# Another order of loads, transposes and vector work around the two halves of an attention stage, before two MLPs

## The reference

```python
B, H, S, D = q.shape                          # 2, 8, 768, 64; block 32, window 16
k_sum = k.reshape(B, H, nb, block, D).max(axis=3)
v_sum = v.reshape(B, H, nb, block, D).mean(axis=3)
scores_l = scale * q @ k^T, kept where |i - j| < window
scores_s = scale * q @ k_sum^T + log(block)
a = softmax over both together
x = a @ concat(v, v_sum)                      # to 1536 tokens x 512
xn = x / rms(x) * rms_g
x = (silu(xn @ w_gate) * (xn @ w_val)) @ w_out     # 512 -> 1536 -> 512
h = x @ w_in ; out = (h - tanh(h)) @ w_out2        # 512 -> 2048 -> 512
```

## Time and profile before

| | us |
|---|---|
| median of 3 runs | 628.69 (628.62 to 629.18) |
| the profiled execution, its own time | 630.96 |
| its span, first to last instruction | 628.9 |
| PE busy in it | 612.5 |
| DVE, ACT, POOL busy | 428.5, 324.1, 171.3 |
| mean granted TensorE clock | 0.995 of full |

### The profile page before, as it was taken

One profiled execution on the slowest core, in us unless ns is written; L12 is line 12 of the kernel. 1 busy time (PEld: TensorE's weight loads), 2 busy tenths in 40 slices (PEclk: granted clock), 3 DMA queues, 4 the chain that ended last, 5 costly groups with the idle time before them and its releaser, 6 DMA issues.

```text
span 628.9 us, 10726 instructions
## 1 busy us (share of the span) xinstructions
PE 612.5 (97%) x3990; PEld 570.6 (91%) x3990; DVE 428.5 (68%) x699; ACT 324.1 (52%) x622; POOL 171.3 (27%) x223
## 2 busy tenths in 40 slices
PE   7889799999999999999999999999999999999997
PEld 7669699999999998889898899999999989898986
DVE  4798567567753449877777689999543597666643
ACT  5676254444433327555555467776332375555542
POOL 4673512021210303322220545662200222222200
PEclk9999989999999999999999999999999999999999
DMA  9998913312311121222222162222323023222102
GB/s 257 189 242 152 185 51 93 92 35 60 93 51 51 52 68 50 69 74 65 75 63 68 45 200 67 68 68 77 91 57 112 0 73 96 67 68 68 33 2 100
DMA packets 96210, 53.90 MB, mean 86 GB/s; under 512 B 33760, under 2 KB 90336, under 8 KB 95968
## 3 DMA queue, kind: packets, MB, share of 16 engines
q1 hardware_dynamic: 95728, 52.44, 32.2%
q10 hardware_dynamic: 432, 0.79, 0.3%
HBM read 50.07 MB, written 3.15 MB: 85 GB/s over the span
## 4 chain that ended last, share of the span: by engine, by line
PE 86%; SPq 10%; DVE 2%; DMA 1%; issue 1%; ACT 1%; DVEq 0%
PE bank L931 11%; PE bank L935 11%; PE bank L933 11%; PE bank L874 10%; PE bank L876 10%; PE bank L875 10%; PE bank L1040 7%; PE bank L1039 7%; PE bank L1038 7%; SPq L497 4%; SPq L447 2%; PE bank L858 1%; PE bank L809 1%; DMA x_raw<-in_moe_w_gate_dram 1%; PE bank L838 1%
## 5 line engine op out<-in xcount | busy, mean ns | idle before, releaser
L1700 DVE TENSOR_TENSOR h_lo<-pd,h_hi 128x384 fp32r<-128x384 f32 x112 | 70.2, 628 | 28.9 <-ACT h_hi L1426 13.9
L1040 PE MATMUL bank<-y_hi,h_lo 128*128 128x512 f32 x192 | 75.5, 393 | 0.0
L1039 PE MATMUL bank<-y_lo,h_hi 128*128 128x512 f32 x192 | 75.4, 393 | 0.0
L1038 PE MATMUL bank<-y_hi,h_hi 128*128 128x512 f32 x192 | 75.3, 392 | 0.0
L698 POOL TENSOR_TENSOR ws_raw<-x_raw 128x256 f32<-128x256 f32 x16 | 12.0, 752 | 209.0 <-PE bank L935 127.5
L874 PE MATMUL bank<-h_hi,z_hi 128*128 128x384 f32 x192 | 64.9, 338 | 0.0
L876 PE MATMUL bank<-h_hi,z_lo 128*128 128x384 f32 x192 | 64.5, 336 | 0.0
L875 PE MATMUL bank<-h_lo,z_hi 128*128 128x384 f32 x192 | 64.5, 336 | 0.0
L1293 ACT CAST h_hi<-pd 128x384 fp32r<-128x384 f32 x48 | 24.8, 516 | 45.5 <-DVE pd L1730 33.6
L1410 ACT COPY part<-bank 128x384 f32<-128x384 f32 x48 | 23.0, 479 | 43.3 <-PE bank L935 42.2
L1040 PEld LDWEIGHTS bank<-y_hi,h_lo 128*128 128x128 f32 x192 | 36.0, 188 | 8.2
(11 more groups left out here) (207 smaller groups left out, 1727.6 us busy)
## 6 DMA issues: line engine op xcount, KB each, us to landing
x_raw<-in_moe_w_in_dram SPq DMA_DIRECT2D x32, 256.0 KB, 3.4
y_raw<-in_moe_w_out_dram SPq DMA_DIRECT2D x32, 256.0 KB, 2.8
x_raw<-in_moe_w_gate_dram SPq DMA_DIRECT2D x24, 256.0 KB, 3.3
y_raw<-in_moe_w_val_dram SPq DMA_DIRECT2D x24, 256.0 KB, 3.3
z_raw<-in_moe_w_out_dram SPq DMA_DIRECT2D x16, 384.0 KB, 3.5
k_rows<-in_k_dram SPq DMA_DIRECT2D x8, 384.0 KB, 5.6
qn<-in_q_dram SPq DMA_DIRECT2D x12, 256.0 KB, 7.1
vw_early<-in_v_dram SPq DMA_DIRECT2D x12, 192.0 KB, 6.1
```

Of the source, the lines that this page charges most:

```text
L1038: nc.tensor.matmul(AB[t][:], a_hi, w_hi, start=begins, stop=False, skip_group_check=True)
L1039: nc.tensor.matmul(AB[t][:], a_hi, w_lo, start=False, stop=False, skip_group_check=True)
L1040: last = nc.tensor.matmul(AB[t][:], a_lo, w_hi, start=False, stop=ends, skip_group_check=True)
L1700: nc.vector.tensor_tensor(dst, full, high.bitcast(f32), ALU.subtract).then_inc(done, 1)
```

## The change

1. **Load queue.** Gate and value columns 2 and 3 (`load_xy(2)`, `load_xy(3)`) and values of tiles 6 and 7 are issued among the queries of batch 1; the two loads of z follow after them.
2. **`blk`.** The 96 rows are numbered by block first, head pair second, and are loaded in two transfers (one for each head of the pairs, 96 partitions with a row of 8 KB) instead of four (one for each pair, 24 partitions with two rows). `gather_sums` takes every fourth column of the identity instead of 24 neighbouring ones.
3. **Tile 0.** On PE `transpose_probs(0, 0)` comes before the three block-sum steps, `transpose_probs(0, 1)` before the third. On ACT each `copy_probs(0, par)` follows its `exp(0, par)`, ahead of the first `means`.
4. **Tile 6.** On DVE `copy_q1(4)` comes before the loop (behind `low_h(0,1,1)`) instead of after `gated(0,2,0)`, and `shift(6, 0)` before `product(0,2,0)` instead of after `low_h(0,2,0)`.

```diff
-    v_b = v.rearrange("b (c h) (n t) d -> b c n h (t d)", h=2, t=BLOCK)
+    v_b = v.rearrange("b (c h) (n t) d -> b h n c (t d)", h=2, t=BLOCK)
...
             sp.wait_ge(means_mm, 1)
-            for c in range(KC):
-                sp.dma_start(blk[c * NBLK:(c + 1) * NBLK, :, :], v_b[1, c]).then_inc(blk_in, 16)
-            for t in range(1, TPB):
-                load_q(TPB + t)
+            for hf in range(2):
+                sp.dma_start(blk[:, hf, :], v_b[1, hf]).then_inc(blk_in, 16)
+            load_q(TPB + 1)
+            load_q(TPB + 2)
+            load_xy(2)
+            load_q(TPB + 3)
+            load_xy(3)
+            load_q(TPB + 4)
+            load_q(TPB + 5)
+            load_values(TPB)
+            load_values(TPB + 1)
             for m in range(2):
                 load_z(m)
-            for i in range(J1 // 2):
-                if i:
-                    load_xy(2 * i)
-                    load_xy(2 * i + 1)
+            for i in range(2, J1 // 2):
+                load_xy(2 * i)
+                load_xy(2 * i + 1)
                 load_values(TPB + i)
...
-            pool.wait_ge(blk_in, 16 * KC)
+            pool.wait_ge(blk_in, 32)
...
-                                            ident[0:KC * NBLK, c * NBLK:(c + 1) * NBLK],
+                                            ident[0:KC * NBLK, c:KC * NBLK:KC],
...
             scores(1)
-            block_sums()
+            transpose_probs(0, 0)
+            block_sums(0)
+            block_sums(1)
+            transpose_probs(0, 1)
+            block_sums(2)
...
             exp(0, 0)
+            copy_probs(0, 0)
             exp(0, 1)
+            copy_probs(0, 1)
             act.wait_ge(means_mm, 1)
             means(vw_early[:, 0], TX).then_inc(means_act, 1)
             copy_q(2)
-            copy_probs(0, 0)
-            copy_probs(0, 1)
...
             low_h(0, 1, 1)
+            copy_q1(4)
...
                 if T == TPB:
-                    copy_q1(4)
+                    shift(T, 0)
                     product(0, j, 0)
                     dve.wait_ge(half_added, ADDS)
                     low_h(0, j, 0)
-                    shift(T, 0)
                     shift(T, 1)
```

More of the change, by code:

```diff
@@ L813, in scores, with block_sums @@
                 last.then_inc(scored, 1)
[L815 to L821, removed]
+            def block_sums(m):
+                if m == 0:
+                    pe.wait_ge(ind_done, 1)
+                pe.wait_ge(v_paired, m + 1)
+                last = nc.tensor.matmul(TX[WIN:KEYS, :], ind[:, m, :], v_rows[:, :, 2 * m * D:(2 * m + 1) * D],
+                                        start=m == 0, stop=m == ROWS // 2 - 1)
+                if m == ROWS // 2 - 1:
+                    last.then_inc(means_mm, 1)
             def gather_sums():
@@ L1127, in _ @@
                     gate(0, 0, 0)
-                transpose_probs(T, 0)
-                transpose_probs(T, 1)
+                if T:
+                    transpose_probs(T, 0)
+                    transpose_probs(T, 1)
                 if T >= 2:
```

## The result

| | before | after |
|---|---|---|
| median | 628.62 (626.82 to 629.18, 5 runs) | 624.05 (623.86 to 624.33, 5 runs) |
| ratio | | 0.9943, interval 0.9922 to 0.9964 |
| profiled execution: time, span | 630.96, 628.9 | 624.17, 622.0 |
| mean granted clock in it | 0.995 | 0.999 |

The kernel is faster, by 4.6 us from median to median. Between the two profiled executions it is 6.9 us of span. The time lies inside the range, near its upper end; the forecast was 7.1 us of gain, less 0.1 for small waits, and 621.7 us.

A forecast was written before the change was run, and what follows sets the result against it. PE was taken as the bound, pausing between batches behind gate column 2's late landing. 6.96 us there plus 0.15 from the first stage made 7.1; 628.69 less that, plus 0.1 for small waits, gave 621.7 us, range 620.3 to 625.0.

The forecast's parts named there:

- The cause: Passage between batches: late gate column 2 delays ACT's split and key copies, DVE's maxima and `copy_q1(3)`, so PE waits 3.56 us.
- The sum: Whole kernel: 6.96 us from the passage plus 0.15 from the first stage, 7.1 us gained.
- The lower clock's part: PE from `gather_sums` to `transpose_probs(6, 0)`: 2.78 us of the 6.96 gain, from the clock staying at full speed.
- the gain taken over whole gives 628.69 - 7.1 = 621.6: Whole kernel: full gain from the profiled execution subtracted from the median of runs, before 0.1 us for small waits.
- the last sentence of the prediction: Least sure: whether unprofiled runs have the whole pause; if the 2.27 us difference lies in it, gain 4.8, time 623.9.
- The range's lower end: Whole kernel: 620.3 us, from the full 0.65 us of the first stage and a `scores(6)` at half.
- POOL in DVE's way: Rival, 0.06: POOL's earlier additions at 53 to 64 us slow DVE, passage some 1 us later, 622.7 us.
- the shorter pause: Rival, 0.14: passage between batches, PE still stops 1 to 2 us and the clock falls, 624.4 to 625.9 us.
- doesn't do what it says: Rival, 0.05: load queue, column 2 still lands after 70 us, the pause stays, 628.2 us.
- the slower case: Rival, 0.05: `blk` lands late and PE stops at `gather_sums`; at half drain rate 11 us later, 639 us.

The follow-up runs named there:

- the two holds: Kernel after, columns 2 and 3 held until batch 1's third query tile is transposed, or until `gate(0,1,1)` is done: 629.75 and 630.36 us.
- The 99 executions: The kernel before, unchanged, timed over five sets: 625.79 to 633.27 us.

## Where the prediction was right, and which step failed

**The cause was right.** The late column, the wait of ACT, the key copies, the maxima, `copy_q1(3)` and PE's pause stood in the forecast as a chain, and the two holds show it as a cause: with the column late again, the pause and the time are back.

**The sum was right for the execution that it was read from.** 630.96 - 7.1 = 623.9 was forecast for it, and the profiled execution after took 624.17. Between the spans are 6.9 us. The first stage and `gather_sums` gave 0.55 us (its end at 70.92 and not 71.47), the stretch to `transpose_probs(6, 0)` 6.84, and 0.4 went back at the two transposes of tile 6. Of the 6.84, 4.18 are the waits, as forecast. The lower clock's part, forecast at 2.78, can be read from `transpose_q1(4)` to `gate(0,2,1)`: 78.02 to 84.08 before and 73.07 to 76.69 after, 2.44 us less. 0.2 us is left over. Term by term: ACT's split at 65.0 (65.06), maxima at 67.65 (67.75), `copy_q1(3)` done at 72.2 (72.35), PE from `gather_sums` to `transpose_probs(6, 0)` 12.47 (12.59), `transpose_probs(6, 1)` from 84.15 (84.28) behind at most 0.3 us of waiting (0.17), the clock up.

**The step that failed** is "the gain taken over whole gives 628.69 - 7.1 = 621.6". The 7.1 us was the price of a pause and of a low clock that this one execution had in full; the 628.69 was the median of other executions, in which part of that pause was missing. Subtracting the whole pause from a median that holds only part of it counts the difference, some 2.3 us, twice: measured were 4.6 us from median to median. The 99 executions bear it out: 51 of them run at a mean clock of 0.999 or more, at a median of 627.53, and 3.5 us, not 7, are to be had from these; from the other 48, at 630.02, it is 6.0. That profiling itself made the 630.96 long is not borne out: the profiled execution of the kernel after took 624.17 beside a median of 624.05, and the profiled one of the kernel before, run again, was the fastest of its twelve. That the 2.27 us were the pause in just those runs is argued from all this; no trace of those runs shows it. The right sum was 630.96 - 7.1 = 623.9, the absolute time of a kernel whose pause is gone; the last sentence of the prediction had it, as its least sure point, and the forecast did not go by it. There was a hint of it beforehand: the profile's time lay above all three runs, and the chain to PE's pause began with the landing of a transfer.

**The range's lower end** was added up wrongly: 621.6 less 0.5 for the rest of the first stage and 0.4 for `scores(6)` is 620.7, not 620.3. Nothing hangs on it.

**Tile 0** was sized at 0.5 us; the trace gives 0.35 (from `scores(1)` to `gate(0,0,0)`, 44.09 - 16.95 against 44.40 - 16.91), since the first means started 0.7 us later and not 0.6 (22.06 against 21.36). Over all seventeen profiles this stretch is 27.48 to 27.50 us in the seven with the old order and 27.14 to 27.16 in nine of the ten with the new one (27.49 in the tenth, the first of the holds). Of it nothing that can be measured reaches the end.

**`blk`.** The forecast left open whether its new form drains faster; it does, by 2.7 us over seventeen profiles (the 3.5 us between the two first profiles hold some scatter). As the sum had it, PE's wait at `gather_sums` was worth 0.2 us. What the forecast missed is the other use of it: every transfer queued behind `blk` comes sooner, so that the kernel with this form and the old order of the queue came to 625.55. The Trainium skill ("SBUF — State Buffer", "Door 1: The DMA port swizzle") had the direction; the forecast made 6 us of it, and the traces 2.7. The 137 GB/s that were said to agree with its estimate of 163 came from one execution: seven of the ten profiles with the old form moved 166 to 199 GB/s in that window, other loads included.

**POOL in DVE's way.** The collisions are there. Two `low_h` that took 0.56 and 0.79 us take longer beside POOL's additions:

```profile
55.76 1.28 DVE L1712 TENSOR_TENSOR h_lo<-pd,h_hi 128x384 fp32r<-128x384 f32 x1
...
59.50 1.60 DVE L1712 TENSOR_TENSOR h_lo<-pd,h_hi 128x384 fp32r<-128x384 f32 x1 [1.13 <-ACT h_hi L1305]
```

They cost 1.5 us of DVE's time and nothing of PE's that shows in its waits. This agrees with the rule cited in the rival; the price of 1 us at the end did not appear.

**The others.** Column 2 landed well before 65, q9 kept nobody waiting, and `blk` was not late: the shorter pause, "doesn't do what it says" and the slower case did not come.

## What to carry to other kernels

A stall that hangs on a transfer's landing is not one number. Take its price from the profiled execution, subtract it from that execution's own time, and hold the result as the time of the changed kernel; if the profiled time lies above the runs, the stall is the first suspect for the difference. Removing such a stall also takes the scatter away: here 623.86 to 624.33 (5 executions) where 625.8 to 633.3 stood (99). When everything behind a slow transfer is late, moving the needed one forward and making the slow one faster are two ways to the same gain, and most of it is there only once.

## What the runs showed of the hardware that was not expected

- The same program's transfers land several us apart from one execution to the next: column 2 was taken up between 66.3 and 74.1 us in four profiles. The start of `gate(0,0,0)` keeps to 1.1 us, and counted from `scores(1)` to 0.02 us.
- With the load into 96 partitions the queue moved 205 to 224 GB/s from 44 to 52 us in seven profiles, with the same bytes into 24 partitions at a time 128 to 199 in ten, other loads included.
- The lower clock came in stretches of 3.4 or 6.8 us: at a stop of PE of 3.5 to 3.7 us in six profiles, and in a seventh at two waits of 1.6 and 1.8 us one after the other and again at one of 2.1. It did not come in the two profiles in which PE's longest wait in the passage was 1.8 us, nor where it was 0.5. The same 3.56 us of pause had 6.8 us of lower clock behind it in the kernel before and 3.4 in the two holds.
